# Experts' second product with w2 stationary, its output turned back, and score pieces of 160 and 416 columns

## What is computed

```python
scores = scale * np.matmul(q, k.transpose(0, 1, 3, 2))      # 2 x 8 heads, 576 x 576
kth = np.partition(scores, -32, axis=-1)[..., -32:-31]
scores = np.where(scores >= kth, scores, -1e9)               # then softmax, times v
h = x @ w_in                                                 # 1152 x 512 @ 512 x 2048
g = h * np.cos(h)
x = g @ w_out                                                # 2048 x 512
expert_idx = np.argmax(x @ w_gate, axis=1)                   # 8 experts, capacity 288
h = np.maximum(np.einsum('ecd,edf->ecf', disp, w1), 0.0)     # 512 -> 1024
y = np.einsum('ecf,efd->ecd', h, w2)                         # 1024 -> 512
out[i] = gate_w[i] * y[expert_idx[i], pos[i]]
```

## Time and profile before

| what | value |
|---|---|
| median of 3 runs | 691.6 us (688.86 to 692.9) |
| the profiled execution, its own time | 688.36 us |
| its span | 686.6 us |
| mean granted TensorE clock | 0.978 |
| PE busy | 636.3 us, 93% |
| DVE busy | 550.3 us, 80% |
| ACT busy | 389.9 us, 57% |
| POOL busy | 375.8 us, 55% |

### The profile page before, as it was taken

The page is one execution under the profiler, slowest core; times in us unless marked ns, Lnnn a source line. Parts: engine busy times, 40 slices in busy tenths (PEclk is TensorE's granted clock), DMA queues, the critical chain, the costliest instruction groups (busy, mean ns, idle before and its releaser), DMA issues.

```text
span 686.6 us, 12837 instructions
## 1 busy us (share of the span) xinstructions
PE 636.3 (93%) x4210; PEld 547.5 (80%) x4210; DVE 550.3 (80%) x1002; ACT 389.9 (57%) x605; POOL 375.8 (55%) x278
## 2 busy tenths in 40 slices
PE   4688988999999999999999999989889999999996
PEld 2576977987987887887988988879677888888884
DVE  5999999989899799898898898433727668777673
ACT  2454675485585485575675674743725645557550
POOL 0769897489588687588597696860500111101111
PEclk9997799999999999999999999999999999999999
DMA  8697000000000000000000000023367555666500
GB/s 325 274 353 289 4 9 5 21 6 8 20 9 5 21 10 5 25 5 4 23 4 17 6 0 17 1 84 147 123 238 314 208 193 195 272 275 248 194 26 15
DMA packets 17790, 68.60 MB, mean 100 GB/s; under 512 B 1998, under 2 KB 6606, under 8 KB 15056
## 3 DMA queue, kind: packets, MB, share of 16 engines
q1 hardware_dynamic: 16000, 63.27, 24.3%
q0 software_dynamic: 1744, 4.73, 2.1%
HBM read 54.33 MB, written 14.45 MB: 100 GB/s over the span
## 4 chain that ended last, share of the span: by engine, by line
PE 61%; DVE 14%; issue 9%; POOL 6%; ACT 5%; DMA 3%; DVEq 1%; POOLq 0%; ACTq 0%; SPq 0%
PE p_o L1092 8%; PE p_a L1129 5%; DVE top L362 5%; PE p_s L1058 4%; DVE arena L365 4%; PE p_t L1074 4%; PE p_b L1129 4%; PE p_b L1157 3%; PE p_b L1159 3%; PE p_b L1158 3%; PE p_s L1300 2%; DVE g_lo L405 2%; PE p_t L1300 2%; PE p_o L1317 2%; PE p_o L1319 2%
## 5 line engine op out<-in xcount | busy, mean ns | idle before, releaser
L362 DVE MAX8 top<-arena 128x8 f32<-128x576 f32 x288 | 203.5, 745 | 16.4 <-ACT arena L779 16.1
L365 DVE MATCH_REPLACE8 arena<-top,arena 128x576 f32<-128x576 f32 x216 | 158.5, 740 | 0.0
L640 POOL TENSOR_SCALAR mask<-arena,top 128x576 f32<-128x576 f32 x72 | 128.2, 1780 | 26.3 <-DVE top L362 18.9
L644 POOL TENSOR_TENSOR arena<-arena,mask 128x576 f32<-128x576 f32 x72 | 103.6, 1439 | 23.8 <-ACT arena L793 13.4
L1092 PEld LDWEIGHTS p_o<-arena,probsT 128*128 128x128 f32 x640 | 87.7, 211 | 14.0 <-ACT probsT L800 10.8
L1092 PE MATMUL p_o<-arena,probsT 128*128 128x65 f32 x640 | 89.7, 292 | 7.0 <-ACT probsT L800 7.0
L800 ACT COPY probsT<-p_t 128x640 f32<-128x640 f32 x72 | 50.4, 701 | 62.7 <-PE p_t L1074 62.4
L1074 PE MATMUL p_t<-ident,arena 128*128 128x128 f32 x360 | 59.0, 299 | 17.9 <-POOL arena L644 17.9
L1074 PEld LDWEIGHTS p_t<-ident,arena 128*128 128x128 f32 x360 | 44.3, 153 | 38.0 <-POOL arena L644 27.5
L779 ACT COPY arena<-p_s 128x576 f32<-128x576 f32 x72 | 44.2, 643 | 48.9 <-PE p_s L1058 48.9
L1058 PE MATMUL p_s<-arena,q_sb 64*128 64x224 f32 (+5 forms) x320 | 62.2, 495 | 7.1 <-DMA arena<-in_kt 4.3
(11 more groups left out here) (174 smaller groups left out, 1285.6 us busy)
## 6 DMA issues: line engine op xcount, KB each, us to landing
arena<-in_w SPq DMA_DIRECT2D x8, 2048.0 KB, 8.8
wff<-in_w SPq DMA_DIRECT2D x8, 2048.0 KB, 9.1
slot_rows<-y_now SPq DMA_DIRECT2D x1, 4626.0 KB, 27.1
wff<-in_w_out SPq DMA_DIRECT2D x1, 4096.0 KB, 19.7
wff<-in_w_in SPq DMA_DIRECT2D x1, 4096.0 KB, 15.3
wff<-slot_rows SPq DMA_DIRECT2D x8, 385.5 KB, 3.6
arena<-in_vones SPq DMA_DIRECT2D x2, 1300.0 KB, 9.1
q_sb<-in_q SPq DMA_DIRECT2D x36, 64.0 KB, 1.9
```

The source lines that it names most:

```text
L362: nc.vector.max(best, src).then_inc(top_step, 1)
L365: nc.vector.match_replace(work[:, a, :], best, src, LOWEST).then_inc(top_step, 1)
L640: nc.gpsimd.tensor_scalar(mask[:], s_sb[:, t, :], top[:, t, TOP_K - 1:TOP_K], None, ALU.is_ge).then_inc(mask_made, 1)
L644: nc.gpsimd.tensor_tensor(probs[:, t % 2, :], probs[:, t % 2, :], mask[:], ALU.mult).then_inc(probs_ready, 1)
```

## The change

**Second product.** It becomes 4 x 8 pairs of matmuls with w2 stationary: for each 128 columns d of the output, and for each of eight hidden groups f, `w2_hi` times high and low activations side by side (384 columns) and `w2_lo` times the high part (192 columns). The two hidden parts are kept side by side in `he_parts` for this. The result has output columns on its partitions. It is handled as units 4 and 5 of the expert: ACT copies the cross part (`copy_cross`), DVE adds it (`sum_unit`) into `y_sum`, and the new `turn_back` transposes it to rows of tokens in `p_oe`, in four transposes of 128 columns for each half h. The half h = 0 is turned after the second product, the half h = 1 after unit 0 of the next expert. The two scalings move from the end of an expert to the middle of the next one.

**Rows and weights.** DVE copies the gate weights and row numbers out of `rows` (`keep`), so that SP loads the rows of an expert first and without a wait for a scatter.

**Scores.** The spots become 96 and 864, and the pieces 160 and 416 columns. Head 0 makes its 160 columns first, and the last piece of head 1 has 160.

```diff
-SPOT = [288 + 512, 512 - 288]
-SPLIT = [512 - 288, 288]
+SHORT = 160
+SPOT = [512 - (S - SHORT), 1024 - SHORT]
...
-                piece_of(0, 0, SPLIT[0]).then_inc(middle_bank_done, 1)
-                piece_of(1, 0, SPLIT[1])
-                piece_of(0, SPLIT[0], S)
+                piece_of(0, S - SHORT, S).then_inc(middle_bank_done, 1)
+                piece_of(1, SHORT, S)
+                piece_of(0, 0, S - SHORT)
 
                 wait(pe, middle_bank_done, 4 * blk + p + 1)
-                piece_of(1, SPLIT[1], S).then_inc(scores_done, 2)
+                piece_of(1, 0, SHORT).then_inc(scores_done, 2)
...
-                wait(sp, he_ready, 4 * E - 4)
+                wait(sp, kept, E - 1)
+                expert_rows(e, j, r)
+                wait(sp, unit_ready, UNITS * E - 2 * UNITS + UP_UNITS)
                 sp.dma_start(w1_raw[j], w1_d[e]).then_inc(w1_in[j], 16)
-                wait(sp, out_sent[j], 16 * NSB * turn)
-                expert_rows(e, j, r)
-                wait(sp, oe_ready, NSB * E - NSB)
+                wait(sp, unit_ready, UNITS * E - UNITS)
                 sp.dma_start(w2_raw[j], w2_d[e]).then_inc(w2_in[j], 16)
...
             def expert(E, j, turn, n, more=True):
+                if not begin:
+                    sum_unit(E - 1, 5, n)
                 low_w2(E, j, 0)
                 low_w2(E, j, 1)
-                sum_he(E, 0, n)
-                for c in range(1, 4):
-                    sum_he(E, c, n)
+                sum_unit(E, 0, n)
+                sum_unit(E, 1, n)
+                low_he(E, 0, n)
+                if not begin:
+                    scale_rows(E - 1, 1 - j, turn - 1 + j, n)
+                for c in range(2, 4):
+                    sum_unit(E, c, n)
                     low_he(E, c - 1, n)
                 low_w2(E, j, 2)
                 low_he(E, 3, n)
                 low_w2(E, j, 3)
                 if more:
                     low_x(E + 1, n)
+                    keep(E + 1, 1 - j, turn + j, n)
                     low_w1(E + 1, 1 - j)
+                sum_unit(E, 4, n)
+                if not more:
+                    sum_unit(E, 5, n)
+                    scale_rows(E, j, turn, n)
...
+            def turn_back(E, h, n):
+                m = NSB * n
+                wait(pe, sum_made, UNITS * E + UP_UNITS + h + 1)
+                if h == 0:
+                    wait(pe, oe_copied, NSB * E)
+                for s in range(NSB):
+                    for d in range(2):
+                        at = P * (2 * h + d)
+                        last = nc.tensor.transpose(p_oe[s][0:n, at:at + P],
+                                                   y_sum[h][:, m * d + n * s:m * d + n * s + n], ident[:])
...
+                    if c == 0 and not (isinstance(E, int) and E % NE == 0):
+                        turn_back(E - 1, 1, n)
...
+                for h in range(2):
+                    wait(pe, sum_made, UNITS * E + UP_UNITS + h - 1)
+                    for d in (2 * h, 2 * h + 1):
+                        for f in range(FC2):
+                            if d == 0 and f % 2 == 0:
+                                wait(pe, he_lo_made, 4 * E + f // 2 + 1)
+                                wait(pe, w2_lo_made, 4 * E + f // 2 + 1)
+                            if f < FC2 - 1:
+                                mm(bank_d[:, 0:2 * m], w2_hi[:, f, cols], both_he, start=(f == 0), stop=False)
+                                mm(bank_d[:, 0:m], w2_lo[j][:, f, cols], high_he, start=False, stop=False)
+                    last.then_inc(unit_ready, 1)
+                turn_back(E, 0, n)
+                if not more:
+                    turn_back(E, 1, n)
```

More of the change, by code:

```diff
@@ L104, in build @@
         he_at = x_at + 2 * KC * SLOTS
-        he_hi = over("he_hi", wff, he_at, [FC2 * SLOTS])
-        he_lo = over("he_lo", wff, he_at + FC2 * SLOTS, [FC2 * SLOTS])
+        he_parts = over("he_parts", wff, he_at, [FC2 * 2 * SLOTS])
         q_sb = sb("q_sb", [P, H // 2, P])
@@ L592, in low_he, with scale_rows, keep @@
                                                ALU.subtract).then_inc(he_lo_made, 1)
+            def scale_rows(E, j, turn, n):
+                wait(dve, out_sent[j], 16 * NSB * turn)
+                for s in range(NSB):
+                    wait(dve, oe_ready, NSB * E + s + 1)
+                    nc.vector.tensor_scalar(oe[j][0:n, s, :], p_oe[s][0:n, :], own_weight[0:n, j, s:s + 1],
+                                            None, ALU.mult).then_inc(oe_copied, 1)
+            def keep(E, j, turn, n):
+                wait(dve, rows_in[j], 16 * (turn + 1))
+                wait(dve, out_sent[j], 16 * NSB * turn)
+                nc.vector.tensor_copy(own_weight[0:n, j, :], rows[j][0:n, :, DM])
+                nc.vector.tensor_copy(own_number[0:n, j, :], rows[j][0:n, :, DM + 1].bitcast(I32)).then_inc(kept, 1)
@@ L605, in expert @@
                     low_x(E + 1, n)
+                    keep(E + 1, 1 - j, turn + j, n)
                     low_w1(E + 1, 1 - j)
[L608 to L612, removed]
+                sum_unit(E, 4, n)
+                if not more:
+                    sum_unit(E, 5, n)
+                    scale_rows(E, j, turn, n)
             low_x(0, ROUNDS[0][1])
+            keep(0, 0, 0, ROUNDS[0][1])
             expert_round(dve, 0, expert)
@@ L618, in _ @@
                 low_x(NE, ROUNDS[1][1])
+                keep(NE, 0, NE // 2, ROUNDS[1][1])
                 expert_round(dve, 1, expert)
@@ L973, in high_w1 @@
                 wait(act, w1_in[j], 16 * (turn + 1))
-                wait(act, he_ready, 4 * E)
+                wait(act, unit_ready, UNITS * E - UNITS + UP_UNITS)
                 for c in range(4):
@@ L1280, in turn_rows @@
                         last.then_inc(xe_ready, 1)
+            def turn_back(E, h, n):
+                m = NSB * n
+                wait(pe, sum_made, UNITS * E + UP_UNITS + h + 1)
+                if h == 0:
+                    wait(pe, oe_copied, NSB * E)
+                pe.sem_inc(tensor_waits, 1)
+                for s in range(NSB):
+                    for d in range(2):
+                        at = P * (2 * h + d)
+                        last = nc.tensor.transpose(p_oe[s][0:n, at:at + P],
+                                                   y_sum[h][:, m * d + n * s:m * d + n * s + n], ident[:])
+                    if h == 1:
+                        last.then_inc(oe_ready, 1)
             def expert(E, j, turn, n, more=True):
@@ L1290, in expert @@
                     wait(pe, w1_lo_made, 4 * E + c + 1)
-                    wait(pe, he_sum_made, 4 * E + c - 1)
+                    wait(pe, sum_made, UNITS * E + c - 1)
                     for f in (2 * c, 2 * c + 1):
@@ L1304, in expert @@
                                 last = mm(bank_f[:, 0:2 * m], w1_hi[:, k, cols], both_x, start=False, stop=True)
-                    last.then_inc(he_ready, 1)
+                    last.then_inc(unit_ready, 1)
+                    if c == 0 and not (isinstance(E, int) and E % NE == 0):
+                        turn_back(E - 1, 1, n)
                 if more:
                     turn_rows(E + 1, 1 - j, turn + j, n)
-                wait(pe, oe_copied, NSB * E)
-                for c in range(4):
-                    wait(pe, he_lo_made, 4 * E + c + 1)
-                    wait(pe, w2_lo_made, 4 * E + c + 1)
-                    for s in range(NSB):
-                        for f in (2 * c, 2 * c + 1):
-                            cols = slice(m * f + n * s, m * f + n * s + n)
-                            a, b = (he_hi[:, cols], he_lo[:, cols]), (w2_hi[:, f, :], w2_lo[j][:, f, :])
-                            mm(p_oe[s][0:n, :], a[0], b[1], start=(f == 0), stop=False)
-                            mm(p_oe[s][0:n, :], a[0], b[0], start=False, stop=False)
-                            last = mm(p_oe[s][0:n, :], a[1], b[0], start=False, stop=(f == FC2 - 1))
-                        if c == 3:
-                            last.then_inc(oe_ready, 1)
```

68 lines of the change are left out of this document (47 added, 21 removed).

## The result

The changed kernel takes 711.5 us (median of 4 runs, 709.4 to 712.8), the kernel before took 690.2 beside it. The ratio is 1.031, 95% interval 1.025 to 1.037: slower, and at the time that was forecast, 712. Its profiled execution took 712.0, with a span of 710.3.

The account below looks back on a forecast made before the run. PE's stream was taken to be the length of an expert. Stalls 4.8, turns 5.6, end 3.2, rows -0.3 and scores -2.0 make 11.3 more, the clock 9 more: 691.6 + 20.3, 712 us, range 699 to 718.

Parts of the forecast that it names:

- The second product: In each expert 32 pairs of matmuls take 9.21 us instead of 11.18, saving PE 1.97, 15.8 in all.
- The wait it meets: In the second product's first sweep PE waits 1.33 and 1.03 for `w2_lo`'s third and fourth quarters: net 4.8 us more.
- The clock: After the new stalls PE's clock falls in 6 of 8 experts, at 1.5 us each: 9 us more.
- Turning back: Eight transposes for each expert, 0.4 us for four, with their sums ready in time: 5.6 us more.
- rival (1): Experts' stalls come but the clock stays at 2.4 GHz or falls once or twice: 703, up to 706; chance 0.30.
- Rival (2): No stalls in the second product, so the kernel is faster: 9.3 us less, 682; chance 0.05.
- rival (4): Turns wait for their sums because DVE is full, 0.5 us more each: 716; chance 0.06.
- The scores: In the attention, shorter last score pieces save 0.22 us eight times and 0.3 at the very first: 2.0 less.
- The end: After the last product, copy, sum, transposes and scaling put the last scatter's issue at 4.8 us: 3.2 more.
- The sum: Whole kernel: 11.3 us more from the other terms and 9 from the clock, 20.3 more in all.

Follow-up runs that it names:

- the quarters early: The changed kernel with DVE making the third and fourth quarters of `w2_lo` earlier: 712.8 us; with `keep` also moved behind `low_w1`, 684.1 us.
- the filled run: The changed kernel with 5 and 3 unread matmuls in PE's two waits of the second product: 709.4 us; with `keep` also behind `low_w1`, 700.7 us.

## Why the prediction was right, point by point

**The second product.** Right. A pair costs 0.28 to 0.29 at full clock. With the quarters early, at a clock of 1.00, the 64 matmuls take 9.8 in most experts, against the 9.2 of the forecast and the 11.2 of before. The 0.6 between lies in the first of the four sweeps, which takes 2.9 where the others take 2.3: PE still waits a little, 0.2 and 0.1, for the low part of h.

**The wait it meets.** Right in mechanism and size: forecast 1.33 and 1.03, in the trace 1.26 and 0.82 of idle time, or 1.4 and 1.0 between two starts beyond a matmul's own 0.1. The product is 11.5 to 11.8 where the clock stays up; forecast 11.7.

**The clock.** Right, and it was the term with the least behind it. It fell in 6 of 8 experts. One fall makes the product 13.35 instead of the 11.77 of expert 6, 1.6, of which the filled run returns 1.4; forecast 1.5. So the earlier trace rows was read the right way: 1.26 and 0.82 of idle time close together act like the 2.07, not like the single 1.29. The 6 itself is luck in part: expert 6 had the same idle time and no fall, with `keep` moved alone all eight had one, and no run shows what decides between the two.

**Turning back.** The price was right: four transposes 0.35 to 0.44 in starts against 0.4, 7.4 measured for 16 more groups. The step before it **failed**: "What they wait for is ready by my layout of DVE: the sum of unit 4 follows the four `low_w1` and ends near 597.0, the second product ends at 598.2". That is 1.2 of slack. In the trace the slack is 0.3, though the fall of the clock put TensorE 1.6 further back. The layout counted `keep` as two small copies. It has a third part, its wait for `out_sent`, and that was 2.6 long. Two things were not laid out: what `keep` waits for, and what stands beside the scatters at their new place. The forecast looked at the loads, found that they keep their triggers or come earlier and that nothing is later there; that holds for w1. But the scatters came to stand on that trigger, and the landing of the second went from 3 to 8.

It did nearly no harm to the number, by luck of arithmetic. TensorE's chain, with stalls and slow clock, is 23.9 from one product to the next, with `keep` moved alone, and the chain through the scatter is 23.8 to 24.5 in four experts of the filled run. Had the clock stayed up, rival (1), the forecast of 703 would have been wrong: that state was made with the filled stalls, and it gave 709.4, while 700.7 came only after `keep` was moved. Rival (2), no stalls, 682, was wrong in the same way: 712.8 as the change stands, 684.1 with `keep` moved. And rival (4) named the right place, a turn that waits for its sum, but gave it 0.5 each, from how full DVE is, and not the 3.3 to 4.4 of a wait behind a DMA that PE had in five turns once its stalls were gone.

**The scores.** The block is 0.23 shorter, forecast 0.22, and by the same one pair in four. The term of 2.0 was under-sized: 3.6 alone, with an interval of 1.9 to 5.4, and 4.9 beside the rest of the change. The steady blocks account for 1.4 to 1.5. What is on top lies outside them, and I can't say how much of it is the pieces' own and how much the chance of a longer or shorter fall of the clock.

**The end.** The last scatter answers the earlier trace rows:

```profile
702.38 0.75 DVE L613 TENSOR_SCALAR h_sb<-p_o,own_weight 96x512 f32<-96x512 f32 x1 [0.65 <-PE p_o L1336]
703.05 0.74 DVE L613 TENSOR_SCALAR h_sb<-p_s,own_weight 96x512 f32<-96x512 f32 x1
704.02 0.92 POOL L794 DMA_INDIRECT out_rows<-h_sb,own_number  x1 [16.49 <-DVE h_sb L613]
705.24 0.92 POOL L794 DMA_INDIRECT out_rows<-h_sb,own_number  x1 [0.30 <-issue]
```

The last product ends near 700.5, and the last scatter is issued 4.8 later, as forecast to the tenth. From there to the end of the span it is 5.1, where the earlier trace rows had 3.8: 1.3 that the forecast left out. Of the 4.5 in all, 2.8 to 3.8 came back with the old product in the last expert, although that product is itself 1.1 longer (11.1 against 10.0).

**The sum.** The changed kernel minus the kernel before is 21.3, forecast 20.3: a term for the scores that was 1.6 to 2.9 too small, an end 1.3 too small, stalls and falls of the clock that make the eight products 15.1 longer and not 13.8, and a wait that was missed and cost next to nothing (0.4).

## What to carry to other kernels

Of every step that is moved, write down what it waits for before what it costs: two tiny copies held up 4.6 us of work and a turn-back, because their wait was for a DMA. When a kernel has an engine that stalls and another chain of nearly the same length, taking one of the two away shows nothing; try both together before giving up a theory. And when small transfers move to another place, look at which large load starts there, and at who waits for the small ones.

## What I had not expected of the hardware

Two short idle stretches of TensorE (1.26 and 0.82, with 0.6 of matmuls between) are followed by 3.4 us at 1.2 GHz in six experts of eight of the changed kernel and in all eight with `keep` moved; filling them there with matmuls that nobody reads, eight of 0.2, made the kernel 11.3 us faster than leaving TensorE idle for the same time. An indirect scatter of 96 rows lands 2.7 to 3.5 us after issue, also when a 2 MB load starts 1.4 behind it; when the load starts 0.2 behind it, it lands after 8.0 to 9.4.
